# A two-block fp32 network with a decay recurrence in front: the decay products as a tree on VectorE, and attention two steps behind

## The reference

```python
mag = sqrt(a_re**2 + a_im**2); scale = minimum(mag, 0.999) / (mag + 1e-6)
a = (a_re * scale, a_im * scale)                    # complex decay, per step t and row d
for t in range(768):                                # batch 4, heads 8, head_dim 48
    S = a[t][:, None] * S + outer(k[t], v[t])       # complex state S (48 x 48), real input
    y[t] = q[t] @ real(S)
x = y, heads side by side                           # 3072 tokens x 384
xn = x / sqrt(mean(x*x) + 1e-6) * rms_g
x = (silu(xn @ w_gate) * (xn @ w_val)) @ w_out      # 384 -> 1536 -> 384
out = softplus(x @ w_in) @ w_out2                   # 384 -> 2048 -> 384
```

## Time and profile before

| | |
|---|---|
| median of 3 runs (lowest to highest) | 1353.83 us (1353.83 to 1358.66) |
| profiled execution: its time, and the span of its instructions | 1369.43 us, 1367.3 us |
| mean granted TensorE clock of the span | 0.946 |
| PE / DVE / ACT / POOL busy, share of the span | 83% / 59% / 46% / 34% |
| DMA | 91.05 MB |

### The profile page before, as it was taken

One profiled execution on the slowest core, in us unless ns is written; L12 is line 12 of the kernel. 1 busy time (PEld: TensorE's weight loads), 2 busy tenths in 40 slices (PEclk: granted clock), 3 DMA queues, 4 the chain that ended last, 5 costly groups with the idle time before them and its releaser, 6 DMA issues.

```text
span 1367.3 us, 19277 instructions
## 1 busy us (share of the span) xinstructions
PE 1132.8 (83%) x5495; PEld 961.8 (70%) x5495; DVE 813.0 (59%) x2300; ACT 631.0 (46%) x1158; POOL 464.5 (34%) x381
## 2 busy tenths in 40 slices
PE   0444348888888888888888888999899999999997
PEld 0444337777777767777777777888788888888886
DVE  6788888788888888988888984112212131212111
ACT  2233333444444444444444432334666666667664
POOL 2144443333333332333333332257333333333332
PEclk9999998899999988999999999999999999999999
DMA  1334442232223233322233223024101010101000
GB/s 37 96 109 127 127 127 75 76 99 76 76 76 99 76 78 76 99 76 76 76 99 76 76 65 87 1 87 122 58 0 47 0 47 1 46 0 46 0 23 24
DMA packets 63086, 91.05 MB, mean 67 GB/s; under 512 B 3985, under 2 KB 52881, under 8 KB 62993
## 3 DMA queue, kind: packets, MB, share of 16 engines
q1 hardware_dynamic: 62992, 89.95, 23.9%
HBM read 60.70 MB, written 29.24 MB: 66 GB/s over the span
## 4 chain that ended last, share of the span: by engine, by line
issue 27%; PE 26%; DMA 18%; DVE 15%; POOL 11%; ACT 1%; SPq 1%; POOLq 0%; DVEq 0%; ACTq 0%
PE gbank L1243 10%; POOL pl L593 9%; DMA rows_scratch<-pk 8%; DMA mm<-rows_scratch 8%; PE ybank L1243 7%; DVE prep L995 5%; DVE prep L871 4%; PE sbank L1260 3%; DMA ytile<-in_w 2%; DVE pk L871 2%; PE xbank L1251 2%; PE xbank L1272 1%; PE xbank L1271 1%; PE xbank L1275 1%; DVE ew L871 1%
## 5 line engine op out<-in xcount | busy, mean ns | idle before, releaser
L1243 PE MATMUL gbank<-xh,slab 128*128 128x512 f32 x1296 | 409.2, 397 | 2.4 <-issue 2.4
L1243 PE MATMUL ybank<-ph,slab 128*128 128x512 f32 x1020 | 340.4, 417 | 4.9 <-ACT ytile L699 4.0
L1243 PEld LDWEIGHTS gbank<-xh,slab 128*128 128x128 f32 x1296 | 244.7, 191 | 52.5 <-issue 2.5
L1243 PE MATMUL gbank<-xl,slab 128*128 128x512 f32 x648 | 255.7, 395 | 0.0
L1243 PEld LDWEIGHTS ybank<-ph,slab 128*128 128x128 f32 x1020 | 202.7, 203 | 46.6 <-issue 5.6
L593 POOL TENSOR_TENSOR pl<-hid,ph 128x512 fp32r<-128x512 f32 x96 | 125.8, 1310 | 268.3 <-ACT ph L808 268.3
L1243 PE MATMUL ybank<-pl,slab 128*128 128x512 f32 x510 | 208.6, 409 | 0.0
L1251 PE MATMUL xbank<-ident,mm 96*128 96x96 f32 x192 | 33.7, 315 | 189.7 <-DMA mm<-rows_scratch 184.5
L1127 DVE SCALAR_TENSOR_TENSOR hid<-gbank,hid 128x512 f32<-128x512 f32 x72 | 49.7, 691 | 214.5 <-ACT hid L799 214.5
L1251 PEld LDWEIGHTS xbank<-ident,mm 96*128 96x128 f32 x192 | 25.5, 182 | 200.6 <-issue 184.0
L538 POOL TENSOR_TENSOR pl<-hid,ph 128x512 fp32r<-128x512 f32 x72 | 96.8, 1344 | 154.7 <-ACT ph L692 154.7
(11 more groups left out here) (138 smaller groups left out, 1831.7 us busy)
## 6 DMA issues: line engine op xcount, KB each, us to landing
rows_scratch<-pk SPq DMA_DIRECT2D x24, 771.0 KB, 5.2
mm<-rows_scratch SPq DMA_DIRECT2D x48, 385.5 KB, 5.2
a_in<-in_a SPq DMA_DIRECT2D x24, 384.0 KB, 6.3
kq_in<-in_kq SPq DMA_DIRECT2D x24, 384.0 KB, 6.1
ytile<-in_w SPq DMA_DIRECT2D x36, 192.0 KB, 2.7
prep<-in_w SPq DMA_DIRECT2D x32, 192.0 KB, 2.6
y_scratch<-ytile SPq DMA_DIRECT2D x7, 768.0 KB, 6.0
v_in<-in_v SPq DMA_DIRECT2D x24, 192.0 KB, 4.7
```

What stands on the lines that cost most here:

```text
L1243: last = pe.matmul(out, slab[:, slot + part, cols], x, start=f, stop=l)
```

## The change

- **Order of the data.** The decays a come from the host with the steps in time order (they were in order of place, then block). The scan runs straight on them: it multiplies with the sum of squares and with the squared scale (SC2) in one instruction, so `m2_of` falls away. The scaled decays are written in order of place, then group and block (`scaled_a`), and the query product reads the scan's result by place.
- **The tree.** Products of pairs of places (p2), of fours (p4) and of the eight (block totals, straight into ga); the four doublings as before, now from the block itself; the frame times gv gives the product at place 7 of every block (`last`), and from there down: place 3 by the upper four, 1 and 5 by pairs, the even ones by single decays.
- **GpSimd.** `s_of`, `m2_of`, `egw_of`, `k_of`, `xl_of` are gone from it. VectorE does the sum (`sum_of`, one unit ahead), both products, keys and queries in four instructions, and `x_low` from PSUM.
- **x.** The gain is multiplied in `x_norm` (one row broadcast to 128 partitions at load), ScalarE takes the high part straight from PSUM, earlier in its list.
- **Attention two steps behind.** LEAD is 7 (n = 4T+7+i), the rows in DRAM have two buffers, mm is loaded by halves of heads: heads 0 to 3 of the next unit already in the step before, heads 4 to 7 at the step's start. Neither waits for the store of the step before. The head has 7 steps; 17 of the 24 steps of the first block have a preparation.
- **The order on VectorE** is cut finer, with small steps of x and of the doublings laid between each other; `decay` and `x_norm` come after `mask`(m,0).

```diff
-LEAD = 6
+LEAD = 7
+LAG = 2
...
+            def load_mm(m, hf, par):
+                after((pk_stored, 16 * (m + 1)), (ys_done[hf], m))
+                heads = slice(hf * HH, (hf + 1) * HH)
                 for z in range(2):
-                    sp.dma_start(mm[z * D:(z + 1) * D, :, :],
-                                 rows_d[z].rearrange("(h d) c -> d h c", d=D)).then_inc(mm_loaded, 16)
...
+            def step(n, m, more, par, w1=None):
                 if m is not None:
                     load_v(m)
-                    load_mm(m)
...
-                    store_pk(n)
+                if more is not None:
+                    load_mm(more, 0, 1 - par)
+                if n is not None:
+                    store_pk(n, par)
...
-            def s_of(n):
-                pool.wait_ge(afront.sem, afront.at("sq", n))
-                pool.tensor_tensor(front[:, 0, :], front[:, 0, :], front[:, 1, :], ALU.add).then_inc(pfront.sem, 1)
...
-            def m2_of(n):
-                pool.wait_ge(aprep.sem, aprep.at("sc2", n))
-                pool.tensor_tensor(W[:, 0, :].rearrange("p (j b i) -> p j i b", j=NJ, i=BK), per_step(front[:, 0:1, :]),
-                                   per_step(prep[:, 9:10, :]), ALU.mult).then_inc(pprep.sem, 1)
...
-            def egw_of(n):
-                pool.wait_ge(dprep.sem, dprep.at("Rnim", n))
-                pool.tensor_tensor(per_step(W), per_step(E), gr_steps(0), ALU.mult).then_inc(pprep.sem, 1)
...
-                act.wait_ge(pfront.sem, pfront.at("s", n))
+                act.wait_ge(s_done, n + 1)
...
+            def sum_of(n):
+                dve.wait_ge(afront.sem, afront.at("sq", n))
+                dve.tensor_tensor(front[:, 0, :], front[:, 0, :], front[:, 1, :], ALU.add).then_inc(s_done, 1)
...
+            def scaled_a(n):
+                tt(A_at[:, 2:0:-1], by_place(a_in[:, :, :]), by_place(prep[:, 3:4, :]).broadcast_to([P, 2, BK, NC]),
+                   ALU.mult, "sc", n)
...
+            def scan(n, j):
+                if j == 0:
+                    dve.wait_ge(aprep.sem, aprep.at("sc2", n))
+                cols = slice(j * CH, (j + 1) * CH)
+                tick(dve.tensor_tensor_scan(PR[:, cols], front[:, 0, cols], SC2[:, cols], 1.0, ALU.mult, ALU.mult))
...
-            def times_a(x, xswap, i, names, out, after, n):
-                tt(e4, x, A5[:, 2:3, :, i, :].broadcast_to([P, 2, NJ, NBK]), ALU.mult, after, n)
-                tt(w4, xswap, A5[:, 0:2, :, i, :], ALU.mult)
-                tt(out, e4, w4, ALU.add, names, n)
...
+            def pairs_re(n):
+                tt(u8, A_even[:, 2:0:-1], A_odd[:, 2:3].broadcast_to([P, 2, BK // 2, NC]), ALU.mult, "an", n)
+            def pairs_im(n):
+                dve.wait_ge(aprep.sem, aprep.at("nim", n))
+                tt(w8, A_even[:, 1:3], A_odd[:, 0:2], ALU.mult)
+            def pairs(n):
+                tt(p2[:, :, :, :], u8, w8, ALU.add, "L1w", n)
...
+            def fours_products(n):
+                tt(u2, p2[:, :, 0::2, :], p2[:, 0:1, 1::2, :].broadcast_to([P, 2, 2, NC]), ALU.mult, "L1", n)
+                tt(w2, p2[:, ::-1, 0::2, :], p2[:, 1:2, 1::2, :].broadcast_to([P, 2, 2, NC]), ALU.mult)
+            def fours(n):
+                tt(p4[:, 0], u2[:, 0], w2[:, 0], ALU.subtract, "L2w", n)
+                tt(p4[:, 1], u2[:, 1], w2[:, 1], ALU.add)
+            def total_products(n):
+                tt(u1, p4[:, :, 0, :], p4[:, 0:1, 1, :].broadcast_to([P, 2, NC]), ALU.mult, "L2im", n)
+                tt(w1, p4[:, ::-1, 0, :], p4[:, 1:2, 1, :].broadcast_to([P, 2, NC]), ALU.mult)
+            def total(n):
+                tt(ga[:, 0, :, 0:NBK], e4[:, 0], w4[:, 0], ALU.subtract, "Tw", n)
+                tt(ga[:, 1, :, 0:NBK], e4[:, 1], w4[:, 1], ALU.add)
...
+            def last_products(n):
+                tt(e4, ga[:, :, :, 1:NBK + 1], scaled[:, 0:1, :].unsqueeze(3).broadcast_to([P, 2, NJ, NBK]),
+                   ALU.mult, "F", n)
+                tt(w4, ga[:, ::-1, :, 1:NBK + 1], scaled[:, 1:2, :].unsqueeze(3).broadcast_to([P, 2, NJ, NBK]),
+                   ALU.mult)
...
+            def last(n):
+                tt(E_7[:, 0], e4[:, 0], w4[:, 0], ALU.subtract, "Gw", n)
+                tt(E_7[:, 1], e4[:, 1], w4[:, 1], ALU.add)
+            def middle_products(n):
+                tt(u1, E_at[:, :, 7, :], p4[:, 0:1, 1, :].broadcast_to([P, 2, NC]), ALU.mult, "Gim", n)
+                tt(w1, E_at[:, ::-1, 7, :], p4[:, 1:2, 1, :].broadcast_to([P, 2, NC]), ALU.mult)
+            def middle(n):
+                tt(E_at[:, 0, 3, :], u1[:, 0], w1[:, 0], ALU.subtract, "D3w", n)
+                tt(E_at[:, 1, 3, :], u1[:, 1], w1[:, 1], ALU.add)
+            def odd_products(n):
+                tt(u2, E_at[:, :, 3::4, :], p2[:, 0:1, 1::2, :].broadcast_to([P, 2, 2, NC]), ALU.mult, "D3im", n)
+                tt(w2, E_at[:, ::-1, 3::4, :], p2[:, 1:2, 1::2, :].broadcast_to([P, 2, 2, NC]), ALU.mult)
+            def odd(n):
+                tt(E_at[:, 0, 1::4, :], u2[:, 0], w2[:, 0], ALU.subtract, "D1w", n)
+                tt(E_at[:, 1, 1::4, :], u2[:, 1], w2[:, 1], ALU.add)
+            def even_products(n):
+                tt(u8, E_odd, A_odd[:, 2:3].broadcast_to([P, 2, BK // 2, NC]), ALU.mult, "D1im", n)
+                tt(w8, E_odd[:, ::-1], A_odd[:, 0:2], ALU.mult)
+            def even(n):
+                tt(E_even, u8, w8, ALU.add, "D0w", n)
+            def query(n):
                 dve.wait_ge(kq_loaded, 16 * (n + 1))
-                dve.wait_ge(dprep.sem, dprep.at("EG", n))
-                for j in range(NJ):
-                    cols = slice(j * CH, (j + 1) * CH)
-                    tick(dve.scalar_tensor_tensor(
-                        out=W[:, 0, cols].rearrange("p (i b) -> p i b", i=BK),
-                        in0=PR[:, cols].rearrange("p (b i) -> p i b", i=BK), scalar=gq[:, j:j + 1],
-                        in1=kq_in[:, 1, cols].rearrange("p (i b) -> p i b", i=BK), op0=ALU.mult, op1=ALU.mult))
-                tt(pk[:, :, :, CH:2 * CH], U.rearrange("p z (j t) -> p z j t", j=NJ),
-                   blocks(W[:, 0, :]).unsqueeze(1).broadcast_to([P, 2, NJ, CH]), ALU.mult, "q2", n)
+                tt(rows(SC2), PR.rearrange("p (j b i) -> p j i b", j=NJ, i=BK), rows(kq_in[:, 1, :]), ALU.mult)
+            def keys(n, z):
+                tt(rows_of(z, 0), by_row(E[:, z, :]), rows(kq_in[:, 0, :]), ALU.mult, "D0", n)
+            def queries(n, z):
+                tt(rows_of(z, CH), by_row(E[:, z, :]), rows(SC2), ALU.mult)
...
+            def x_low(x, par, col):
+                dve.wait_ge(xh_done, x + 2)
+                dve.tensor_tensor(x_columns(xl, par, col), sbank[:, 0:NJ * CH].rearrange("p (j t) -> p j t", j=NJ),
+                                  x_columns(xh, par, col).bitcast(F32), ALU.subtract).then_inc(xl_done, 1)
...
```

More of the change, by code:

```diff
@@ L90 @@
 ACT_FRONT = "sq ln r0 r02"
-ACT_PREP = "w2 sc2 nim e6 lnp g0"
-POOL_FRONT = "s"
-POOL_PREP = "m2 EGw K"
+ACT_PREP = "w2 sc2 nim lnp g0"
 DVE_PREP = (
[L95 to L98, removed]
[3 rows of a table added]
 )
@@ L539, in lo, with tile @@
                                    ALU.subtract).then_inc(lo_done, 1)
-            def step(n, x, par=0, col=0, T=None, i=0, w1=None, last=False):
-                if n is not None:
-                    m2_of(n)
-                if w1 is not None:
-                    w1_lo(w1)
-                if T is not None:
+            def tile(T, last=False):
+                for i in range(UT):
                     if last and i:
@@ L567, in step @@
                     lo(T, 3 * i + 2)
[L568 to L576 removed]
                 if last:
                     w2_lo_of(F1 - 1)
[L580 to L589 removed]
+            with pool.Fori(0, F1) as f:
+                w1_lo(f)
+            with pool.Fori(0, NT - 1) as T:
+                tile(T)
+            tile(NT - 1, last=True)
             def lo2(T, f):
@@ L952, in prep_frame, with after_sums, end_1, end_2 @@
+            def after_sums(n, d):
+                dst = gb if d in (1, 4) else ga
+                tt(dst[:, 0, :, 0:NBK], e4[:, 0], w4[:, 0], ALU.subtract, f"w{d}", n)
+                tt(dst[:, 1, :, 0:NBK], e4[:, 1], w4[:, 1], ALU.add)
+            def end_1(n):
                 dve.wait_ge(aprep.sem, aprep.at("g0", n))
                 tt(gt[:, :], g0[:, :], pend, ALU.mult)
+            def end_2(n):
                 tt(gt[:, :], gt[:, :], g0[:, :], ALU.mult, "g1", n)
+            def end_3(n):
@@ L1081, in step @@
                 if n is not None:
-                    prep_frame(n)
+                    last(n)
+                if x is not None:
+                    x_low(x, par, col)
+                if n is not None:
+                    middle_products(n)
+                    middle(n)
                 if T is not None:
                     p_of(T, 3 * i + 2)
+                if n is not None:
+                    odd_products(n)
+                    query(n)
+                    odd(n)
                 if m is not None:
@@ L1087, in step @@
```

(15 more changed lines are left out.)

384 lines of the change are left out of this document (184 added, 200 removed), and 3 rows, old and new, of the table DVE_PREP.

## The result

The changed kernel takes **1304.89 us** (median of 4 runs, 1300.64 to 1310.46) beside 1356.24 us for the kernel before in the same comparison (4 runs, 1353.83 to 1361.01): ratio 0.962, interval 0.957 to 0.967. It is faster, by half of what was forecast (51 us of 101.7), and the time lies 5 us above the range (1210 to 1300). The profiled execution took 1304.69 us, its span is 1302.9 us, its mean granted clock 0.959 (0.946 before).

The account below looks back on a forecast made before the run. TensorE and VectorE were taken to wait in turn on rows stored to and loaded from DRAM. Steps -107.9, attention step +26.6, next one -7.8, head -12.6 gave -101.7, 1252 us after subtracting 15.6 profile excess; range 1210 to 1300.

Parts of the forecast that it names:

- the strided reads: VectorE's scaled decays and query: one more element time per strided element, 0.8 + 0.4 = 1.2 us a step.
- drowning in strided reads: Rival: stride makes decays 11 and query 5 us on VectorE, +15 a step, some 1600 us; chance 0.05.
- VectorE's own step: VectorE, per step: 25.3 us of own work plus port and y_copy waits, 29.2 us.
- the port: VectorE beside GpSimd's three lo a step: 1.05 us at the scans, 1.2 at even places, 0.3 at the middle one.
- mm no longer waits: TensorE's key transposes: the 4.4 us a step of waiting for mm goes, through two steps of distance.
- y_copy's wait: VectorE's state_add(m,0) waits 1.3 us a step for ScalarE's y_copy.
- the clock term: TensorE before xt_of: idle 1.2 to 2.6 us, clock falls in one step of three, +0.8 us a step.
- a fall in every step: Rival: the clock falls in each step, 26.6 + 1.2 + 5.2 = 33 us a step, 1303 us; chance 0.13.
- the slack argument: TensorE has 1.4 us of slack, so after a fall the next gap is short and the clock holds.
- the border: TensorE's clock: no fall after 1.43 us idle, a fall after 2.65 us; the forecast gap lies between.
- The rest of the span: After the steps with a preparation: one more attention step, +26.6 us, and the next no longer waiting for rows, -7.8.

Follow-up runs that it names:

- e3_pe_order: Changed kernel with TensorE's gate product of 3i+2 (9 matmuls) moved ahead of the transpose of x: 1250.84 us, 0.919.
- e7: Kernel with the tree and mm loaded by halves, but LEAD 6, both halves loaded behind the store: 1292.61 us, 0.953 against the kernel before.
- e8: Kernel before with only the second step of distance (LEAD 7, two row buffers, mm by halves): 1373.27 us, 1.012.
- e4_filler: Changed kernel with nine thrown-away matmuls (2.0 us) ahead of the transpose of x, nothing else moved: 1262.18 us, 0.926.
- e2_x_early: Changed kernel with x_norm and the small steps of x ahead of mask(m,0) and decay on VectorE: 1263.34 us, 0.929.
- e1_p_late: Changed kernel with p_of(3i+2) moved behind odd places and query on VectorE: 1300.88 us, 0.956.
- e5_s_pool: Changed kernel with the sum of squares back on GpSimd, one unit ahead, behind lo(3i): 1344.40 us, 0.986.

## Why the prediction was half right

**Right: the strided reads.** Scaled decays 1.64 us (forecast 1.76), query 0.91 (0.96; 0.89 in the step shown), so the rival of drowning in strided reads is out. In the head, where little else runs, they are 1.54 and 0.83, in place of 0.96 and 0.56 without the stride. So reading in steps of 32 bytes cost 0.7 to 0.8 ns more per element, about seven tenths of the element time that I took, and the second strided input next to nothing more. By the rule of the Trainium skill, SBUF — State Buffer, Specifications, that each crossing into a new 16-byte line is penalised, the trace agrees.

**Near: VectorE's own step.** It was forecast at 29.2 us with its waits. By e3_pe_order's clean steps it is 27.8, 1.4 less, but the ring of 28.6 stands above it, which the prediction didn't have. That the 29.2 is near the 29.0 us which a step takes without the clock's share (below) is luck.

**Right: the port.** The third scan beside `lo` took 1.51 instead of 0.40, 1.1 us more (forecast 1.05); the key rows beside the other `lo` 1.97 for two (550.82), and 1.03 in the head without it (27.23), 0.9 more (forecast 1.2, at the even places).

**Right: mm no longer waits,** the decay neither. But the cause that I gave was wrong. I credited the two steps of distance (4.4 us of waiting each step). The tree with mm by halves takes nearly all of the wait away (e7). In its usual step the rows leave VectorE 1.9 us after TensorE's step starts instead of 3.0, and from there to the first transposes of the keys pass 8.4 to 10.0 us instead of 11.2 to 12.9, as they need only the first half of mm. The distance, without the tree, moves the wait to the mask (e8).

**Right in place, off in size: y_copy's wait,** 0.7 us in short steps and 2.4 after a long fall (forecast 1.3). With the gap filled it is 0.7 in every step where it occurs, so what lies above that is a consequence of TensorE's clock.

**The step that failed: the clock term.** The prediction put it as: "TensorE has 1.4 us of slack (2.6 - 1.2) to give, so after a fall VectorE is held up 2 to 3.6 us, the next gap is short, and the clock holds. I take a fall in one step of three: +0.8". The first half holds: the gap is 2.3 us, inside its 1.2 to 2.6, and after a fall VectorE is held up, at p_of(3i+2) for 4.2 instead of 2.5 us. The conclusion doesn't follow. VectorE walks its list in order, so being held up moves x_norm by the same amount as the matmuls, and the gap returns in full in the next step: 16 waits in 16 steps, 37.3 us together. A fall in each step is 2.5 us by e4_filler instead of 0.8: (2.5 - 0.8) x 17 = 29 of the 32 us that the steps miss. (By the granted clock of 0.91 it is 2.9 of the 31.9 us, which leaves 29.0; e4_filler still loses 0.3.) The prediction had this as a rival (a fall in every step, 33 us, 1303 us), named its evidence, and gave it 0.13 on the strength of the slack argument. Its fall of 5.2 us was too large, since 10 of the 17 falls cost only 1.7 us, and its base of 26.6 + 1.2 = 27.8 was short of the ring's 28.6. That its 1303 us lies so near the measured 1304.89 is luck: a step 1.1 us too long makes up for the 13 us of the medians and the rest. Nor does the border hold that the prediction drew between 1.43 and 2.65 us of idle time: in e2_x_early the clock fell behind 0.77.

**A wait it had not named.** It looked for what would hold VectorE and named only y_copy. p_of(3i+2) stands right ahead of it in the ring, behind outputs and gate and value on TensorE. Had I followed both engines once round from x_norm to the next x_norm, the ring and the fixed gap could have been added up from rows 5, 7 and the orders.

**The bounds.** The rest of the span came to 3.9 us less gain than the forecast's +26.6 - 7.8. By the traces the two steps without a preparation take 27.0 us each (before: one of 33.5), +20.5 where the forecast had +18.8; the other 2 us lie at the border at which the table is cut and behind these steps. And 13.4 us of the miss are no mechanism at all. What the profiled execution of before had above its median was its own. It should have widened the range by 13 us instead of being subtracted.

**Left open.** Why the same gap of 2.3 us is followed by 3, 7 or 10 us at the lower level; what all engines wait for at the border of the loop over pairs of tiles; and why, with the tree, the gap is 2.3 us and a step 31.9 at the distance of two, where the gap is mostly 1.5 to 2.0 and a step 31.1 at one.

## What to carry to other kernels

Where two engines wait for each other in turn, walk the ring once round in both lists and add it up: a stall in it gives no slack to the next round, because an engine that works in order passes the delay on. Look for what the late engine's partner could do of its own next work while it waits; one product moved ahead of a wait was worth as much here as a rewrite of the preparation. Before giving a wait a cause (the transfer, the distance), ask what would end last if it were gone: here it was a mask at the same time. And one profiled execution is one sample: keep its distance to the median as an uncertainty, not as a constant to subtract.

## What was unexpected in the hardware

- Nine thrown-away matmuls of 2.0 us a step made the program 3.7% shorter (0.926 / 0.962, each ratio against its own runs of the kernel before): the clock went from 0.91 to 0.99 in the steps.
- The same idle time of 2.1 to 2.3 us was followed by a lost 1.7, 3.4 or 5.2 us, and in two steps of e1_p_late by none (one of them the step of 28.8 us). In e2_x_early 0.8 us was enough for a fall.
- An instruction of 1.07 us on GpSimd (e5_s_pool) lengthened the step by 2.2 us, by way of the port, VectorE's path to x_norm and the clock. The Trainium skill, SBUF — State Buffer, Who interferes with whom, has the port that VectorE and GpSimd share as an exclusive lock; the third scan (1.51 for 0.40 beside `lo`) agrees.
- At the border of the loop over pairs of tiles TensorE stood still for 1.9 to 2.5 us with nothing in the profile that it waited for (2.4 before, 2.0 after, 2.5 in e4_filler).
